# Window attention, gated mixing and a wide MLP on one core: copies of turned probabilities moved ahead of exponentials, and one tile's fetches moved ahead of another's

## What is computed

```python
# attention: a window of n_local = 96 keys back, and n_global = 8 global keys
scores = scale * q @ k.T + bias;  scores[~keep] = -1e9
a = exp(scores - max);  a = a / (sum(a) + 1e-9);  x = a @ v
# gated mixing of tokens
h = relu(x @ w_in);  u, v = split(h);  v_n = layer_norm(v)
x = (u * (w_spatial @ v_n + b_spatial)) @ w_out
# low-rank mixing of tokens and an MLP of width 2048
u = x + (x.T @ U @ V).T;  out = u + relu(u @ w_ch1) @ w_ch2
```

## Time and profile before

| | us |
|---|---|
| median of 3 runs | 531.95 (531.86 to 531.96) |
| the profiled execution | 533.03 |
| its span | 531.1 |
| TensorE busy | 516.4 (97%) |
| VectorE busy | 278.4 (52%) |
| ScalarE busy | 187.5 (35%) |
| GpSimd busy | 136.2 (26%) |

### The profile page before, as it was taken

The page is one execution under the profiler, slowest core; times in us unless marked ns, Lnnn a source line. Parts: engine busy times, 40 slices in busy tenths (PEclk is TensorE's granted clock), DMA queues, the critical chain, the costliest instruction groups (busy, mean ns, idle before and its releaser), DMA issues.

```text
span 531.1 us, 7551 instructions
## 1 busy us (share of the span) xinstructions
PE 516.4 (97%) x2638; PEld 405.3 (76%) x2638; DVE 278.4 (52%) x767; ACT 187.5 (35%) x470; POOL 136.2 (26%) x166
## 2 busy tenths in 40 slices
PE   6899999999999999999999999999999999999996
PEld 4566666577777788888888888888888888888885
DVE  5759898787776458775422564341255522111112
ACT  5758786766666433332420101021010121001010
POOL 7854603222222011381599920000000000000000
PEclk9999999999999999999999999999999999999999
DMA  7896756636743024292133300020000002000002
GB/s 157 202 204 134 145 107 142 135 76 120 132 74 106 12 40 64 34 193 50 39 118 120 118 2 1 1 79 1 0 1 0 1 0 81 0 1 0 1 0 84
DMA packets 72186, 36.89 MB, mean 69 GB/s; under 512 B 57424, under 2 KB 66896, under 8 KB 72144
## 3 DMA queue, kind: packets, MB, share of 16 engines
q1 hardware_dynamic: 51024, 20.10, 18.6%
q0 software_dynamic: 4512, 14.29, 9.8%
q10 hardware_dynamic: 16608, 1.97, 2.6%
HBM read 32.15 MB, written 3.15 MB: 66 GB/s over the span
## 4 chain that ended last, share of the span: by engine, by line
PE 83%; DVE 7%; issue 3%; ACT 2%; DMA 2%; SPq 1%; DVEq 0%; ACTq 0%
PE ps L1464 72%; PE ps L1429 4%; PE ps L1485 3%; PE ps L1513 2%; DVE sc L1045 2%; DMA qk_odd<-in_k 1%; PE ps L1602 1%; ACT pr L695 1%; SPq L410 1%; DVE q_turned L987 1%; DMA n_raw<-in_n_local 1%; DVE pr L1060 1%; PE ps L1612 1%; DVE small L1117 0%; DVE xT_lo L1018 0%
## 5 line engine op out<-in xcount | busy, mean ns | idle before, releaser
L1373 DVE SCALAR_TENSOR_TENSOR hT_lo<-ps,hT_hi 128x512 fp32r<-128x512 f32 x48 | 33.2, 691 | 167.5 <-ACT hT_hi L904 167.5
L904 ACT ACTIVATE hT_hi<-ps 128x512 fp32r<-128x512 f32 x48 | 28.7, 598 | 223.2 <-PE ps L1464 223.2
L695 ACT ACTIVATE pr<-sc,small 128x256 f32<-128x256 f32 (+1 forms) x96 | 46.2, 483 | 34.1 <-DVE small L1045 34.0
L1464 PE MATMUL ps<-win_hi,xT_hi 128*128 128x512 f32 x96 | 39.9, 416 | 0.4 <-issue 0.4
L1045 DVE CUSTOM_DVE_ANT_0 sc<-ps,bias 128x256 f32<-128x256 f32 (+1 forms) x96 | 34.9, 399 | 10.2 <-PE ps L1485 8.7
L1214 DVE STREAM_TRANSPOSE ys<-tokens 32x128 f32<-32x128 f32 x128 | 38.7, 302 | 1.8
L1464 PE MATMUL ps<-win_hi,xT_lo 128*128 128x512 f32 x96 | 37.7, 393 | 0.0
L1464 PE MATMUL ps<-win_lo,xT_hi 128*128 128x512 f32 x96 | 37.5, 391 | 0.0
L1464 PE MATMUL ps<-uT_hi,w1a_hi 128*128 128x512 f32 x96 | 37.5, 390 | 0.0
L1464 PE MATMUL ps<-uT_hi,w1a_lo 128*128 128x512 f32 x96 | 37.4, 389 | 0.0
L1464 PE MATMUL ps<-w2a_lo,hT_hi 128*128 128x512 f32 x96 | 37.4, 389 | 0.0
(11 more groups left out here) (161 smaller groups left out, 1108.9 us busy)
## 6 DMA issues: line engine op xcount, KB each, us to landing
w_raw<-in_moe_w_ch POOLq DMA_DIRECT2D x16, 512.0 KB, 4.1
vn<-in_v SPq DMA_DIRECT2D x12, 256.0 KB, 3.7
out<-ys SPq DMA_DIRECT2D x11, 256.0 KB, 2.2
wsp<-in_moe_w_spatial POOLq DMA_DIRECT2D x28, 96.0 KB, 3.5
qk_late<-in_q SPq DMA_DIRECT2D x24, 112.0 KB, 3.8
qk_late<-in_k SPq DMA_DIRECT2D x24, 112.0 KB, 3.6
vp<-in_v SPq DMA_DIRECT2D x10, 224.0 KB, 4.6
w_raw<-in_moe_w_in POOLq DMA_DIRECT2D x4, 512.0 KB, 5.2
```

The costliest lines, as they stand in the source:

```text
L695: act.activation(pr[:, k % 3, e, 0:w], sc[:, k % 2, e, 0:w], ACT.Exp, bias=nmax[:, k % 2, e:e + 1], scale=-1.0, accum_out=sums[:, k % 3, e ...
L904: act.activation(hT[0][:, n % 2, :], h1_ps(n), ACT.Relu).then_inc(s["hT_hi"], 1)
L1373: dve.scalar_tensor_tensor(hT[1][:, n % 2, :], h1_ps(n), 0.0, hT[0][:, n % 2, :], ALU.max, ALU.subtract).then_inc(s["hT_lo"], 1)
L1464: ins = pe.matmul(o, lhsT[a], r[c], start=first_of_bank and (a, c) == (0, 0), stop=last and (a, c) == (1, 0))
```

## The change

SP: for the third tile (tile = 2) the loop now ends behind load_v(1), and load_v(2) is issued for tile = 3, behind load_qk(3) and ahead of load_v(3). ScalarE: in the loop of units 0 to 29, for k >= 10, probs_out(k) is called ahead of exps(k + 2) and normal_half(k + 1), where it was called behind them. Units 0 to 9 and 30 to 47 keep their order.

```diff
+SOON = 10
...
                 if tile == 2:
                     load_v(1)
+                    continue
+                if tile == 3:
+                    load_v(2)
                 if tile == 4:
...
                     t, q = (k - LAG) // NP, (k - LAG) % NP
                     if t >= 1 and q == 1:
                         gv_hi(0, t - 1)
+                    if k >= SOON:
+                        probs_out(k)
                     exps(k + 2)
                     normal_half(k + 1)
...
-                    probs_out(k)
+                    if k < SOON:
+                        probs_out(k)
```

## The result

The changed kernel takes 538.36 us (median of 4 runs, 537.91 to 538.84) against 531.96 for the kernel before in the same job: 1.2% slower, a ratio of 1.0119 with a 95% interval of 1.0107 to 1.0131, or +5.7 to +7.0 us. The forecast was 536.9, +4.98, in a range of 534.8 to 540.0. Its profiled execution took 538.49 us with a span of 536.7.

A forecast was written before the change was run, and what follows sets the result against it. TensorE's own work was taken to bound the attention units. Pauses of 7.94 less 1.55 for the fetches and 1.41 handed back gave +4.98 on the median 531.95: 536.9 us, range 534.8 to 540.0.

The forecast's parts named there:

- The bound: Attention stage, first 104 us: TensorE's own work bounds the units, period 3.21 us; a microsecond lost moves the end by one.
- Part 2, the waits of x_hi: Units 12, 16, 20, 24, 28: exponentials and norm_half stand behind x_hi's wait for the values product; five pauses, together 7.94 us.
- What comes back: The pauses give VectorE time, so the later idle rows at 82.94, 94.93 and 103.65 us vanish: about 1.41 us returned.
- Part 1, the fetches: Fourth tile's queries and keys fetched earlier, so the stall around 40 us before unit 10 goes: a gain of 1.55 us.
- The moved fetches hurt what they pass: Rival, 12%: the fourth chunk or values come over 3.6 us late, unit 9 waits, part 1 gives nothing: 538.5 us.
- Nothing is handed back: Rival, 10%: VectorE stays late, or the late exponentials make it so: 538.3 us, up to 540.
- more is handed back: Rival, 7%: pauses of 1.4 us each and 2.0 us returned: 535.4 us.
- the other side: Rival, 7%: exponentials in units 12 to 28 could not start before x_hi's end anyhow, so the wait costs nothing: 530.1 us.
- The clock: Rival, 2%: TensorE's clock falls in the five new pauses, one unit each at 1.2 GHz, adding 16 us: about 553 us.
- no row shows it: Argument against the clock rival: the profile shows a full clock through the idle 1.4 us around 40 us.
- Full throughout: The prediction's reading of the profile before: TensorE's clock is full over all forty slices.

The follow-up runs named there:

- the next execution: The kernel before, unedited, run again for its profile: 531.73 us, with VectorE waiting 0.99 us for the keys.
- copies-only kernel: The kernel before with only ScalarE's new order from unit 10, load_v(2) staying behind load_v(1): 538.01 us against 531.97, ratio 1.0115.
- fetches-only kernel: The kernel before with only the fetches moved, ScalarE keeping its old order: 532.01 us against 531.97, ratio 0.9998.
- the second run of the kernel with x_hi left behind: Changed kernel, but x_hi taken out of probs_out and left behind norm_half, run again: 531.43 us against 532.18 for the kernel before, ratio 0.9986.
- two-pauses: Changed kernel with ScalarE's new order from unit 21 instead of 10: 533.68 us against 532.32 for the kernel before, ratio 1.0026.
- the 540.01 us execution: Changed kernel with only x_hi ahead of the exponentials, copies of turned probabilities in their old place, run again for its profile: 540.01 us.

## Why the prediction was right, and where its terms were off

**The bound.** TensorE's own work bounds the units, and what is lost in the loop stays lost. Right: T(30), the first unit behind the loop, moved by 5.50 us, and the span by 5.6.

```profile
108.50 0.60 PE L1429 MATMUL ps<-ident,pr 128*128 128x128 f32 x4
114.00 0.60 PE L1436 MATMUL ps<-ident,pr 128*128 128x128 f32 x4
```

**Part 2, the waits of x_hi.** Right in place, number and size. The working gave 4.82 us from T(12) to T(13); it was 4.75, and 4.23 for unit 24 (93.74 - 89.51) where it gave 4.29 (the start of T(24) is 89.51). Against the undisturbed periods the five pauses come to about 1.55 (three times), 1.44 and 1.54, together 7.63 instead of 7.94. Two kernels settle that x_hi and not the copy makes them: without x_hi ahead no pause is left, with x_hi alone ahead they are all there.

**What comes back.** Right: the stalls at units 23 and 27 and before the loop's last scores are gone. With only units 24 and 28 changed, exactly the two stalls behind the first pause are gone. From T(12) to T(30) it is 60.81 us before and 66.89 after, 6.08 more; with pauses of 7.63 that leaves 1.55 handed back, where 1.41 was booked.

**Part 1, the fetches.** This is the term that was mis-sized. The mechanism is as described: the keys are there when wanted and nothing that they pass comes late. The gain of 1.55 us was read from one execution, which had the longest landing of four. In the other three the idle time was 0 to 0.42 us, and the cost on the path 0 to 0.48. The prediction had the hint in its own numbers: that execution took 1.08 us more than the median, and the sum put the whole difference on the median without asking where the 1.08 lay. The cost of 1.55 less the 0.48 of the next execution, 1.07, is that much. With 0.3 in place of 1.55 and 7.63 in place of 7.94 the sum is 531.95 + 7.63 - 0.3 - 1.41 = 537.9 for the changed kernel, which took 538.36, and without the fetches 538.2 for the copies-only kernel, which took 538.01. The changed kernel's two executions with a mean clock of 0.997 took 538.49 and 538.84, the other two 537.91 and 538.22, so a good part of the missing 0.5 us goes with the clock. That the fetches are worth 0.3 is inferred from the profiles; the timed runs can't tell it from nothing.

**The range.** The time lies in the stated range of 534.8 to 540.0, but just over the forecast's own range, 535.2 to 538.3, to which the prediction gave its 60%. The total alone would have spoken for two rivals (538.5 and 538.3) rather than for the forecast; it is the rows that decide against them.

**The rivals.** "The moved fetches hurt what they pass" gave 538.5, near the measured time, for the wrong reason: part 1 did give almost nothing, but no weight chunk or value came late. The fourth chunk's last piece was split at 32.62 + 0.78 = 33.40 where it was at 33.27, with the DMA share at 1.10 in 20-24 instead of 0.35:

```profile
32.62 0.78 POOL L527 TENSOR_TENSOR win_lo<-w_raw,win_hi 128x256 fp32r<-128x256 f32 x1
```

So of the rule of the Trainium skill on the turns of the queues (DMA: Bandwidth & Descriptors, "Queues, rings and completion order") no price shows here: 0.13 us, of which 0.10 is the later start of this execution, under a cover of 3.6. "Nothing is handed back" (538.3, as near as that) fell with the 1.55 us that came back, "more is handed back" with the same number, and the other side with the five pauses.

**The clock.** The rival was given 2% and a price of 16 us for five falls. No fall follows the pauses of 1.4 to 1.5 us in the profile of the changed kernel, nor in any other profile of this case; it has one at 22 us, behind 1.19 us without work in a stretch of sparse work, and its price is about 0.93 us. The "no row shows it" of the prediction was true of the one profile it had, and too strong: that profile has the wait of 1.18 us too, and in three of the ten profiles with such a wait the clock fell behind it. "Full throughout" was too strong as well: by the durations TensorE ran at half pace until about 16 us there. Neither touches the sum. The Trainium skill warns of idle gaps between bursts (TensorE: Matmul & The Clock Gate, "Why this matters for your kernels"), but of longer ones than those here. The measurement differs: the pause of 2.01 us was followed by a fall in one profile of three.

## What to carry to other kernels

Before a call is moved ahead on an engine that works in order, list every instruction inside it with the semaphore that it waits for. A copy that could run early took with it, every fourth time, one whose input is made late in the same unit, and all that the next unit needed stood behind it. And where the profiled execution takes longer than the median, look for the difference among the stalls before one of them is booked as a gain: a wait for a DMA in one profile is a sample, not a rate.

## What the runs showed of the hardware

- The landing of the same eight fetches (112 KB each) in the same order of issues made VectorE wait 2.12, 0.99, 0.81 and 0 us in four executions of the same fetch order (in the last it asked some 0.5 us later).
- TensorE's granted clock may fall to 1.2 GHz behind the same gap in one execution and not in another: behind 1.2 us at 21 us it fell in the profiles of the changed kernel, of the fetches-only kernel and of the second run of the kernel with x_hi left behind, and not in seven others with the same wait, two of the kernel before among them; behind 2.01 us in one of three profiles. Behind 1.4 to 1.7 us in denser work it fell in none. A fall cost 0.9 us of TensorE's time at 22 us and 1.5 us at 107 us.
- There is no sign that the moved fetches make the low clock more frequent: a mean clock of 0.997 or less is on record for 14 of 59 executions of the kernel before (24%), and for 11 of 46 (24%) of the changed, fetches-only, x_hi-left-behind and two-pauses kernels. With idle matmuls in the wait it is 0 of 16.
- TensorE works at half pace at the start of every profile, with the granted clock shown as 1.00 (four score products took 1.23 us, later 0.70). The full pace came by 17 us in twelve profiles and after 20 us in two; in the kernel before the later change put T(7) back by 0.52 us.
- When the pace rose goes with the fall at 22 us. In the three profiles with a fall, the score products at 15.5 us already took 0.70 us. Of the seven with the same wait and no fall, one had 0.70 there (the 540.01 us execution) and six had 0.76 to 1.23. Three falls are few, and why the two go together is open.
